# Token order for finished blocks: 32x32 block transposes on VectorE and SBUF-to-SBUF transfers in place of TensorE transposes and ScalarE copies

## What is computed

```python
# q, k, v: (4, 4, 1088, 32); 8 features per factor
q_p, k_p = phi(q), phi(k)                    # outer product of two projections, 64 features
kv = einsum('bhsf,bhsd->bhfd', k_p, v);  z = sum(k_p, axis=2)
x = (q_p @ kv) / (q_p @ z + 1e-6)            # then (token, 128)
xn = x / sqrt(mean(x * x) + 1e-6) * rms_g
y = (silu(xn @ w_gate) * (xn @ w_val)) @ w_out          # d_ff = 1536
logits = y @ phi                                         # 32 slots
d = softmax(logits, over tokens);  slot_input = d.T @ y  # the dispatch
slot_out = relu(slot_input @ w1) @ w2                    # per expert, 4 slots each
out = softmax(logits, over slots) @ slot_out
```

## Time and profile before

| | us |
|---|---|
| median of 3 runs | 324.19 |
| lowest and highest run | 322.28, 324.56 |
| the profiled execution | 323.99 |
| its span | 321.9 |
| PE busy | 292.0 (91%) |
| DVE busy | 224.3 (70%) |
| ACT busy | 168.2 (52%) |
| POOL busy | 29.3 (9%) |

### The profile page before, as it was taken

The page is one execution under the profiler, slowest core; times in us unless marked ns, Lnnn a source line. Parts: engine busy times, 40 slices in busy tenths (PEclk is TensorE's granted clock), DMA queues, the critical chain, the costliest instruction groups (busy, mean ns, idle before and its releaser), DMA issues.

```text
span 321.9 us, 6390 instructions
## 1 busy us (share of the span) xinstructions
PE 292.0 (91%) x2555; PEld 236.3 (73%) x2555; DVE 224.3 (70%) x439; ACT 168.2 (52%) x317; POOL 29.3 (9%) x44
## 2 busy tenths in 40 slices
PE   2348399999999999999999999999999999998985
PEld 1348287878878788887888787888888777896463
DVE  4668959687677767685876768676767666975244
ACT  1325345566545555655565475566556655557422
POOL 1002755010000001000100100010001000000000
PEclk9998779999999999999999999999999999999995
DMA  7998003920000100000009900000000000000007
GB/s 200 230 237 269 3 2 82 416 91 0 2 0 3 65 3 0 0 3 0 2 6 286 298 2 0 2 0 0 3 0 3 0 2 0 0 2 2 1 5 278
DMA packets 18878, 20.09 MB, mean 62 GB/s; under 512 B 3488, under 2 KB 15520, under 8 KB 18848
## 3 DMA queue, kind: packets, MB, share of 16 engines
q1 hardware_dynamic: 18176, 19.29, 20.2%
q10 hardware_dynamic: 672, 0.39, 0.5%
HBM read 17.45 MB, written 2.23 MB: 61 GB/s over the span
## 4 chain that ended last, share of the span: by engine, by line
PE 81%; DVE 9%; SPq 3%; DMA 3%; issue 2%; ACT 1%; POOL 0%; DVEq 0%; ACTq 0%
PE bank L858 75%; DMA area<-in_k 3%; PE bank L890 2%; SPq L308 2%; PE bank L931 1%; PE bank L911 1%; DVE area L680 1%; DVE area L628 1%; DVE hl L715 1%; PE bank L1102 1%; DVE hid L709 1%; DVE logit L777 1%; DVE comb L777 1%; ACT woh L501 0%; SPq L314 0%
## 5 line engine op out<-in xcount | busy, mean ns | idle before, releaser
L709 DVE TENSOR_TENSOR hid<-bank,silu 128x512 f32<-128x512 f32 (+1 forms) x108 | 71.3, 660 | 65.1 <-PE bank L858 51.2
L473 ACT ACTIVATE silu<-bank 128x512 f32<-128x512 f32 (+1 forms) x108 | 61.9, 573 | 80.1 <-PE bank L858 79.1
L715 DVE TENSOR_TENSOR hl<-hid,hh 128x512 fp32r<-128x512 f32 (+1 forms) x108 | 70.3, 651 | 0.1
L481 ACT ACTIVATE hh<-hid 128x512 fp32r<-128x512 f32 (+1 forms) x108 | 64.7, 599 | 0.8 <-PE bank L858 0.6
L858 PE MATMUL bank<-hh,woh 128*128 128x512 f32 (+1 forms) x108 | 43.8, 406 | 0.4 <-DVE hl L715 0.4
L858 PE MATMUL bank<-xh,wgh 128*128 128x512 f32 (+1 forms) x108 | 42.8, 396 | 0.4 <-DVE xl L688 0.4
L858 PE MATMUL bank<-xh,wvl 128*128 128x512 f32 (+1 forms) x108 | 41.1, 381 | 0.0
L858 PE MATMUL bank<-hh,wol 128*128 128x512 f32 (+1 forms) x108 | 41.1, 381 | 0.0
L858 PE MATMUL bank<-xh,wgl 128*128 128x512 f32 (+1 forms) x108 | 41.1, 380 | 0.0
L858 PE MATMUL bank<-xh,wvh 128*128 128x512 f32 (+1 forms) x108 | 41.0, 380 | 0.0
L858 PE MATMUL bank<-hl,woh 128*128 128x512 f32 (+1 forms) x108 | 40.9, 379 | 0.0
(11 more groups left out here) (137 smaller groups left out, 367.6 us busy)
## 6 DMA issues: line engine op xcount, KB each, us to landing
area<-in_moe_w SPq DMA_DIRECT2D x1, 4096.0 KB, 14.4
area<-in_moe_w SPq DMA_DIRECT2D x8, 512.0 KB, 6.3
y_nat<-in_v SPq DMA_DIRECT2D x4, 512.0 KB, 7.1
q_in<-in_q SPq DMA_DIRECT2D x16, 128.0 KB, 2.6
out<-area SPq DMA_DIRECT2D x8, 256.0 KB, 2.2
area<-in_k SPq DMA_DIRECT2D x14, 128.0 KB, 6.2
area<-in_moe_w_gate SPq DMA_DIRECT2D x1, 768.0 KB, 12.5
area<-in_moe_w_val SPq DMA_DIRECT2D x1, 768.0 KB, 13.9
```

Of the source, the lines that this page charges most:

```text
L473: act.activation(silu[n][:, 0:w], gate_b[n][:, 0:w], ACT.Silu).then_inc(s_silu_ready, 1)
L481: act.activation(hh[m % NH][:, 0:w], hid[m % 2][:, 0:w], ACT.Copy).then_inc(s_hh_ready, 1)
L709: dve.tensor_tensor(hid[n][:, 0:w], val_b[n][:, 0:w], silu[n][:, 0:w], ALU.mult).then_inc(s_hid_ready, 1)
L715: dve.tensor_tensor(hl[m % NH][:, 0:w], hid[m % 2][:, 0:w], hh[m % NH][:, 0:w].bitcast(F32), ALU.subtract).then_inc(s_hl_ready, 1)
```

## The change

For blocks 0 to 7 the way of the finished tokens into `y_nat` is another. DVE takes over a part: at c = 3 of block j + 1 it transposes `yT` in blocks of 32x32 into a new buffer `yZ` (in place of the unused `xT_raw`). In `yZ` each 32x32 block is transposed, but lies where it lay. SP then moves the blocks to their places by sixteen transfers of 32 partitions x 4 runs of 128 bytes, 16 KB each, within SBUF. The transpose of block j waits until the transfers of block j - 1 have landed (`s_y_stored`, 256 counts a block), and ACT's next copy into `yT` waits for the transpose. PE's four transposes, ACT's copy and PE's waits for it go; block 8 keeps the old way. The dispatch waits for the transfers of all of blocks 0 to 7.

```diff
@@ SP @@
+            def tokens_of(j):
+
+                sp.wait_ge(s_yZ_ready, j + 1)
+                for Q in range(P // NS):
+                    for x in range(P // NS):
+                        sp.dma_start(y_blk[x * NS:(x + 1) * NS, j, :, Q * NS:(Q + 1) * NS],
+                                     yZ[Q * NS:(Q + 1) * NS, :].rearrange("p (t x d) -> p t x d", t=HT, d=NS)[:, :, x, :])\
+                            .then_inc(s_y_stored, 16)
+
             for b in range(1, B):
+                if b > 1:
+                    tokens_of(2 * b - 4)
+                    tokens_of(2 * b - 3)
                 sp.wait_ge(s_qT_ready, 2 * b)
...
+            for j in range(4, NB):
+                tokens_of(j)
@@ ACT @@
             def layer_T(j):
                 act.wait_ge(s_out_done, C * j + C)
+                if later(j):
+                    act.wait_ge(s_yZ_ready, j)
...
-                    if c == 7 and not first:
-                        layer_tokens(j - 1)
@@ DVE @@
+            def finished_blocks(j):
+                dve.wait_ge(s_yT_ready, j + 1)
+                if later(j):
+                    dve.wait_ge(s_y_stored, YD * j)
+                dve.transpose(yZ, yT[:, :]).then_inc(s_yZ_ready, 1)
...
+                    if c == 3 and not first:
+                        finished_blocks(j - 1)
@@ PE @@
-                if later(jn - 2):
-                    pe.wait_ge(s_y_ready, jn - 2)
...
-                for t in range(nt):
-                    ins = pe.transpose(bank_c[:, t * P:(t + 1) * P], yT[:, t * P:(t + 1) * P], ident[:, :])
-                ins.then_inc(s_y_ps, 1)
+                if last:
+                    for t in range(nt):
+                        ins = pe.transpose(bank_c[:, t * P:(t + 1) * P], yT[:, t * P:(t + 1) * P], ident[:, :])
+                    ins.then_inc(s_y_ps, 1)
...
             pe.wait_ge(s_dispa_ready, 1)
-            pe.wait_ge(s_y_ready, NB - 1)
+            pe.wait_ge(s_y_stored, YD * NB)
```

More of the change, by code:

```diff
@@ L92, in fused_attention_moe @@
         x_at, x_sq, x_n = (area4[:, n * W:(n + 1) * W].rearrange("p (t d) -> p t d", t=HT) for n in range(3))
-        qT, xT_raw = (area4[:, n * W:(n + 1) * W] for n in (3, 4))
+        qT, yZ = (area4[:, n * W:(n + 1) * W] for n in (3, 4))
         b_sb = sb("b_sb", [P, HT * H, R])
@@ L228, in fused_attention_moe @@
         s_y_ready = sem("y_ready")
+        s_yZ_ready = sem("yZ_ready")
+        s_y_stored = sem("y_stored")
+        YD = 16 * (P // NS) * (P // NS)
         s_logit_ready = sem("logit_ready")
@@ L461, in layer_tokens @@
                 nt = width(j) // P
-                act.wait_ge(s_y_ps, j + 1)
+                act.wait_ge(s_y_ps, 1)
                 act.activation(y_blk[:, j, 0:nt, 0:P], bank_c[:, 0:width(j)].rearrange("p (t d) -> p t d", d=P), ACT.Copy)\
@@ L919, in finish @@
                     pe.wait_ge(s_logit_ready, NB)
-                    pe.wait_ge(s_y_ready, NB)
                 else:
@@ L1071, in _ @@
             pe.wait_ge(s_disp_ready, 1)
-            pe.wait_ge(s_y_ready, NB + 1)
+            pe.wait_ge(s_y_ready, 1)
             dispatch(NA, NT, part_b[1], NA, NT).then_inc(s_part_ps, 1)
```

## The result

The changed kernel is slower: a median of 328.36 us (327.15 to 329.71, 4 runs) against 323.87 (322.28 to 324.56), a ratio of 1.0143 with a 95% interval of 1.0107 to 1.0179. The page of its profiled execution (329.19 us, span 327.0) in three lines: busy time, the granted clock in 40 slices of 8.2 us, and the small transfers that came in.

The account below looks back on a forecast made before the run. PE was taken to bound the kernel, busy throughout each whole 29.20 us block. Gains of 2.0 us less 1.0 lost at the dispatch took 1.0 off, giving a 323.2 us median, own range 321.8 to 324.8.

Parts of the forecast that it names:

- the clock drops: Rival at the dispatch: after a wait of some 4 us PE falls to its lower clock, up to 3.4 us more, 329.6; chance 0.06.
- the slow issue: Rival on SP: each transfer issue takes 0.67 us, like L361, adding 3.0 us at the end, 326.2; chance 0.18.
- full gain: Rival in the blocks and at the end: x_n isn't late, or transfers are quicker; 320.9 to 321.8 us; chance 0.11.
- five signs of being wrong: Block period 28.8 or 29.2; issues 0.6 us or more; landing above 3; clock fallen after 294; DVE idle for q_in.
- I take 0.465 from start to start: SP's issue pitch for the sixteen transfers: block 7's last issue starts 15 x 0.465 = 7.0 us after the first.
- point of decision for q: SP's queue order: q of batch 2, behind block 1's transfers, comes in time up to 0.89 us per issue.
- 0.41 - 0.23 = 0.18 us for x_n: PE, blocks 1 to 6: coming 0.41 earlier against 0.23 slack, it waits 0.18 us for x_n, gaining 0.23 per block.
- DVE's transpose: Added at c = 3: 0.71 us for 128x512, fitting the 0.78 us wait before hid; upper bound 1.10.
- Block 8: Half-wide block: the transpose delays hid by some 0.6 us, costing PE's gate matmuls 0.2 and leaving 0.2 of 0.41.
- Landing: End of block 7's transfers: the last lands 2.2 us after its issue starts, as the output stores do, at 295.4.
- the rival of a slow landing: At the end: the last transfer lands after 8.9 us instead of 2.2, as 128-byte-run loads did; 329.9 us; chance 0.08.
- The queue's rival: SP's queue backs up: 1.15 us per issue, 10.3 us more at the end, q 4 us late twice; 333 to 339; chance 0.08.

Follow-up runs that it names:

- experiment on forms: Changed kernel with blocks 0 to 6's sixteen transfers each in another form, data to wrong places; one execution at 331.05 us, time not compared.
- the second experiment: Changed kernel with the dispatch's wait cut in two, block 7's transfers awaited only ahead of the last 6 tiles; 324.81 us, ratio 1.0061.
- filling work: Changed kernel plus eighteen 128x512 matmuls whose result nothing reads, on PE ahead of the wait for the transfers; 326.58 us, ratio 1.0084.
- The strided transpose: Changed kernel with DVE's transpose reading and writing by the strides of q's, tokens in wrong order; 328.37 us.
- the seven-block version: Changed kernel with block 7 alone brought to token order by PE's transposes and ACT's copy again; 321.20 us, ratio 0.9922.

## Why the prediction was wrong, point by point

The forecast was 323.2 us and "within 1%", a little faster than before. The time lies inside the range, but on the other side of the kernel before: it is that of the rival "the clock drops", which contains the slow issue, with most of the rival "full gain" on top. Three of the five signs of being wrong that the prediction named came: a period of 28.8, issues of 0.6 us, a fallen clock after 294.

**The issue was mis-sized, and that turned the sign.** The step that failed is "I take 0.465 from start to start", with its term "15 x 0.465 = 7.0": it measured 10.5 us (284.05 to 294.6), at 0.64 us from start to start and 0.8 more for the one slow issue. I took the pitch from loads out of device memory, because the shapes agreed and four or more of them stood in a row. The row with SBUF as its source, L361 at 0.67, was read as a slower case of the same thing and made a rival with 0.18. The experiment on forms shows that for these transfers the shape does not matter and the source does. With 10.5 in place of 7.0 and all other measured terms but the clock, the prediction's sum is 323.2 + 3.5 - 0.4 (landing) - 0.95 (gain) = 325.4, slower than before. In its point of decision for q (0.89 us per issue) it was right: q of batch 2 was issued at 130.08 and DVE's transpose of it started at 137.40, back to back with the work ahead of it.

**The clock was a rival with 0.06 and came.** It was made to depend on a wait of some 4 us, from an issue at 0.67; the second experiment shows it behind a wait of 2.16 us. Its price of up to 3.4 us measured 2.45 in the traces and 1.5 to 1.8 between the medians with and without filling work. The prediction gave the slow issue without the clock 0.18 and with it 0.06. As the slow issue by its own sum makes PE wait some 4 us, it should have been the other way round, and the sum for a slow issue should have had the clock in it. With the 2.45 the sum above is 327.8; the median was 328.4.

**The gain was mis-sized the other way.** The forecast had 2.0 us; the trace shows 2.95, nearly all of 8 x 0.41. The step that failed here is that PE itself waits "0.41 - 0.23 = 0.18 us for x_n". x_n was indeed late for the weight loader, and by that amount, in the changed kernel's timelines of weight loads and of PE in block 3:

```profile
155.93 0.44 PEld L936 LDWEIGHTS bank<-ident,area 128*128 128x128 f32 x4 [0.19 <-DVE area L699]
...
155.78 0.40 PE L885 MATMUL bank<-xh,wvl 128*128 128x512 f32 x1
156.01 0.60 PE L936 MATMUL bank<-ident,area 128*128 128x128 f32 x4
```

But the matmul started at 156.01, 0.23 us after the one ahead of it, which is the steady pace. In the kernel before, the loader had started on x_n at 156.35 and the matmul at 156.57, 0.22 us later; now they stand 0.08 apart. The loader's lead took up the wait: the deadline here is the matmul's start, not the start of its weight load. The strided transpose confirms it: the loader waited 0.28 us, the lead was down to 0.01, and PE lost 0.06.

**DVE's transpose** was priced at 0.71 us and took 0.70, from the slope of the rows of q_rem and the 64-column ones; it fitted in front of hid, which still waited 0.15 us for PE:

```profile
147.35 0.70 DVE L714 STREAM_TRANSPOSE area<-yT 128x512 f32<-128x512 f32 x1
148.21 0.69 DVE L734 TENSOR_TENSOR hid<-bank,silu 128x512 f32<-128x512 f32 x1 [0.15 <-PE bank L885]
```

**Block 8** was to lose 0.2 us on PE to the transpose. PE's gate matmuls at c = 6 started at 284.91 instead of 284.80, 0.1 us late; the step was right in kind and half as large.

**Landing** was put at 2.2 and measured 1.8. The rival of a slow landing fell, and the 128-byte runs were not what made the 8.9 us of the earlier trace rows: in the experiment on forms the sixteen transfers of the same runs out of device memory, in a queue with nothing else, landed after 1.8 us too.

```profile
y_nat<-in_q SPq DMA_DIRECT2D x16, 16.0 KB, 1.8
```

In "DMA: Bandwidth & Descriptors", Specifications, the Trainium skill has runs under 512 bytes miss line rate. The same page, "Why small descriptors are slow (HBM only)", says that transfers within SBUF don't suffer the penalty of small descriptors. The 1.8 us within SBUF agree with that section, but as device memory gave the same 1.8 at 16 KB, the landing does not tell the two apart.

**The queue's rival** has a sum that doesn't close: 323.2 + 10.3 and twice 16 x (1.15 - 0.89) = 4.2 us for a late q is 342, not 339. It did not come: the issues of one block took 10 to 11 us.

**In steady state the transfers hid**, as forecast: DVE never waited for a store, and the seven-block version shows no cost of 112 transfers.

From trace to trace the terms give -2.95 + 4.55 + 2.45 = +4.05 us; the medians differ by 4.5. The 0.4 us between them is less than executions of one kernel differ by.

## What to carry to other kernels

A transfer that replaces on-chip work is cheap while a later block covers it and dear for the last one: price the last block by (number of issues) x (pitch) + landing against the moment of its first use, and leave the last block to the old way or start it earlier. Take the pitch only from a row with the same source and destination memories and a like shape (out of device memory alone this kernel's loads show 0.42 and 0.61 us), and where the trace has none, as here, measure one series first: one small experiment did it. And price a pause of PE with the slower clock behind it, not by its length alone.

## What the runs showed of the hardware that was not expected

- An issue on SP costs 0.60 us from SBUF to SBUF and 0.43 from device memory to SBUF, for the same shape in series of sixteen, and the size hardly matters (4 KB 0.59, 64 KB 0.64).
- A pause of PE of 2.16 us, behind 3.2 us of dispatch matmuls, was followed by the lower clock level, which came as PE started again; 1.0 us was lost to it. In the pause of 4.51 us the level fell some 1.3 us in, and 2.45 us were lost.
- Work whose result nobody reads, put into the pause, kept the clock up and made the kernel 1.5 to 1.8 us faster than idling did.
- A weight load that waited 0.19 us for its operand cost PE nothing, and one that waited 0.28 us cost 0.06.
- A block transpose on DVE of 128x512 float32 takes 0.70 us between contiguous rows and 1.12 with 16-byte steps.
